# Attention, routing and eight experts on one Trainium2 core: zero products first, shorter routings, a new order on VectorE and ScalarE, and search tables of their own for two experts

## The reference, cut to what matters

```
attention   B=4, H=8, S=768, D=64; each chunk of 32 queries sees 16 keys to the left, its own 32,
            8 to the right and 8 memory keys; softmax over these 64; times the values
x           attention output as 3072 rows of 512
logits      x @ w_gate                      # 3072 x 8
routing     flat logits in descending order; a token goes to the expert of its largest logit whose
            count is still below cap = 384; so every expert gets exactly 384 tokens
for e in 8: h = relu(x[mask] @ w1[e]);  y[mask] = h @ w2[e]      # 512 -> 1024 -> 512
tail        z = y @ w_in (512 -> 1024); u = z * softmax(z); u centred, scaled by 1/std and g_ln;
            out = u @ w_out (1024 -> 512)
```

## Time and profile before

| | us |
|---|---|
| median of three runs | 782.75 |
| lowest and highest run | 779.54, 783.77 |
| the profiled execution | 780.36 |
| its span, first to last instruction | 778.6 |
| PE busy, share of the span | 704.8 (91%) |
| DVE / ACT / POOL busy | 541.3 / 327.2 / 314.7 |

### The profile page before, as it was taken

One profiled execution on the slowest core, in us unless ns is written; L12 is line 12 of the kernel. 1 busy time (PEld: TensorE's weight loads), 2 busy tenths in 40 slices (PEclk: granted clock), 3 DMA queues, 4 the chain that ended last, 5 costly groups with the idle time before them and its releaser, 6 DMA issues.

```text
span 778.6 us, 17877 instructions
## 1 busy us (share of the span) xinstructions
PE 704.8 (91%) x7092; PEld 626.8 (81%) x7093; DVE 541.3 (70%) x1957; ACT 327.2 (42%) x537; POOL 314.7 (40%) x241
## 2 busy tenths in 40 slices
PE   6799973299979999999999999999999999999992
PEld 5688862298878989798889898989898888889882
DVE  4376756887788688868886978688868877631240
ACT  1255536141365136513651474147315631572270
POOL 3011108582276138514751574158316821672011
PEclk9699985599999999999999999999999999999997
DMA  8699994340232033103310331033113301330001
GB/s 346 205 356 371 337 379 179 100 158 2 82 95 82 28 95 120 58 27 99 119 56 28 122 122 55 33 99 113 55 54 108 108 31 55 109 109 28 0 14 40
DMA packets 24924, 89.07 MB, mean 114 GB/s; under 512 B 3360, under 2 KB 3360, under 8 KB 24864
## 3 DMA queue, kind: packets, MB, share of 16 engines
q0 software_dynamic: 13056, 46.14, 18.0%
q1 hardware_dynamic: 11808, 42.17, 14.5%
HBM read 75.71 MB, written 12.58 MB: 113 GB/s over the span
## 4 chain that ended last, share of the span: by engine, by line
PE 67%; DVE 11%; POOL 8%; issue 5%; DMA 5%; ACT 3%; SPq 0%; POOLq 0%; DVEq 0%; ACTq 0%
PE banks L544 18%; PE banks L546 16%; PE banks L545 16%; POOL wl L1360 5%; DMA raw<-w,w_idx 4%; PE banks L475 3%; PE banks L432 3%; PE banks L456 3%; PE bank L442 2%; DVE z L1174 2%; PE bank L467 2%; POOL raw L1354 2%; PE banks L573 1%; PE banks L557 1%; DVE hits L995 1%
## 5 line engine op out<-in xcount | busy, mean ns | idle before, releaser
L1360 POOL TENSOR_TENSOR wl<-raw,wh 128x1024 fp32r<-128x1024 f32 x60 | 146.1, 2435 | 20.0 <-ACT wh L758 18.6
L1354 POOL DMA_INDIRECT raw<-w,w_idx x60 | 64.7, 1079 | 158.7 <-DVE w_idx L1089 121.5
L544 PE MATMUL banks<-xh,wh 128*128 128x384 f32 x256 | 90.9, 355 | 3.6 <-POOL wl L1360 3.4
L544 PE MATMUL banks<-hh,wh 128*128 128x384 f32 x256 | 90.5, 354 | 0.0
L546 PE MATMUL banks<-xh,wl 128*128 128x384 f32 x256 | 87.0, 340 | 0.0
L545 PE MATMUL banks<-xl,wh 128*128 128x384 f32 x256 | 86.8, 339 | 0.0
L546 PE MATMUL banks<-hh,wl 128*128 128x384 f32 x256 | 86.4, 338 | 0.0
L545 PE MATMUL banks<-hl,wh 128*128 128x384 f32 x256 | 86.3, 337 | 0.0
L758 ACT ACTIVATE wh<-raw 128x1024 fp32r<-128x1024 f32 x60 | 63.3, 1056 | 42.8 <-DMA raw<-w,w_idx 42.5
L544 PE MATMUL banks<-wout_h,uh 128*128 128x512 f32 x192 | 78.7, 410 | 0.2
L544 PE MATMUL banks<-win_h,yh 128*128 128x512 f32 x192 | 77.2, 402 | 0.0
(11 more groups left out here) (202 smaller groups left out, 1622.1 us busy)
## 6 DMA issues: line engine op xcount, KB each, us to landing
unit<-qk_in SPq DMA_DIRECT2D x24, 768.0 KB, 6.2
vr<-v_in SPq DMA_DIRECT2D x24, 520.0 KB, 5.0
x_rows<-x_keep SPq DMA_DIRECT2D x20, 256.0 KB, 5.0
prep_first<-w_in SPq DMA_DIRECT2D x4, 512.0 KB, 6.8
x_rows<-x_sb SPq DMA_DIRECT2D x4, 256.0 KB, 4.3
prep_first<-w_out SPq DMA_DIRECT2D x2, 512.0 KB, 8.8
prep_rest<-w_out SPq DMA_DIRECT2D x2, 512.0 KB, 10.2
raw<-w,w_idx POOLq DMA_INDIRECT x60, 4.2
```

The costliest lines, as they stand in the source:

```text
L544: nc.tensor.matmul(bank, stat_h, mov_h, start=first, stop=False)
L1354: gp.indirect_dma_start(stage(s, c), None, table, bass.IndirectOffsetOnAxis(ap=w_idx[:, c % WCH:c % WCH + 1], axis=0))\
L1360: gp.tensor_tensor(wl[:, c % WCH, :], stage(s, c), wh[:, c % WCH, :].bitcast(F32), ALU.subtract)\
```

## The change

It has five parts.

1. **Start.** SP issues unit 0 first and `wg` and `gain` behind it. TensorE multiplies a cleared 128x128 block with a cleared 128x512 block three times (`WARM`) before its loop, as soon as VectorE has cleared `pr[:, 1]`.
2. **Routing.** `place` is shortened for all experts: a scan that starts at 1000 and a triangular matrix with -1000 on its diagonal take the place of three operations; position and place are whole numbers, so that the third comes by a shift and the place by a mask. The work on `keep` and `M` goes into a new function `close` behind `write_ids`. `write_ids` is one reduction. For expert 0, positions are split in six spans of 64: `hot_b` has 1536 elements in place of 3072, and `token_ids` has 48 products in place of 24. `choose(0)` names the weight rows last, and the table `flips` is made inside the levels. Only six of the eight weight pieces are split ahead of expert 0; GpSimd makes the last two after expert 0's own weights.
3. **z stage on VectorE and TensorE.** The order is `choose, place, max_z(0), write_ids, close, best_open, weigh(0), max_z(1), begin_search, count, max_z(2), search, row_low`; for expert 0, `row_low` comes ahead of `max_z(2)`. TensorE takes `token_ids` after (3,1) and `best_T` after (5,0). ScalarE takes the exponential of z tile 0 one group earlier and its centring right behind it.
4. **h stage on ScalarE.** The last exponential, and the weight conversions 4 and 5, change places: the exponential of tile 2 comes in group 3, the conversions one group later, conversion 7 behind the last `uT_high`.
5. **Tables.** Two rounds instead of one are taken ahead of an expert's h groups; nothing stands at (7) of the first o group. Expert 0's and expert 1's searches have tables of their own, and VectorE's order (`COUNTS...`) is kept apart from TensorE's (`ROUNDS...`).

The diff, cut to its core:

```diff
-ROUNDS = rounds_of([[2]], [[2], [2], [3], [], [3], [3], [3], []], [[2, 7], [4]], [[0, 5], [2, 7], [4], [1, 6]])
-ROUNDS_FIRST = rounds_of([[0, 0]], [[2], [2], [2], [3], [3], [3], [3], [3]], [[], []], [[1, 5], [1, 5], [1, 5], [3]])
+ROUNDS = rounds_of([[0, 5]], [[2], [2], [3], [], [3], [3], [], [1]], [[2], [4]], [[0, 5], [2, 7], [4], [1, 6]])
+ROUNDS_FIRST = rounds_of([[0, 0]], [[2], [2], [2], [3], [3], [3], [3], [3]], [[], []], [[4], [1, 5], [1, 5], [1, 6]])
+ROUNDS_SECOND = rounds_of([[0]], [[], [2], [3], [], [3], [3], [], [1]], [[2], [0, 5]], [[0, 4], [1, 5], [1, 5], [1, 6]])
...
+COUNTS = rounds_of([[0, 5]], [[2], [2], [3], [], [3], [3], [3], []], [[2], [4]], [[0, 5], [2, 7], [4], [1, 6]])
...
+            pe.wait_ge(probs, 1)
+            blank = pr[:, 1, :, :, :].rearrange("p h a w -> p (h a w)")
+            for _ in range(WARM):
+                nc.tensor.matmul(PT_PS[:, :], blank[:, 0:P], blank, start=True, stop=True)
...
             def token_ids(f):
                 pe.wait_ge(hot_ready, f + 1)
+                parts = 2 if f == 0 else 1
+                wide = P // parts
                 for t in range(NT):
-                    mm = nc.tensor.matmul(TOT[:, 16:22], hot_b[:, t, :], rhs_id[:, t, :],
-                                          start=(t == 0), stop=(t == NT - 1))
+                    for a in range(parts):
+                        mm = nc.tensor.matmul(TOT[wide * a:wide * a + wide, 16:16 + 2 * TILES], hot_b[:, t, 0:wide],
+                                              rhs_id[:, t, TILES * a:TILES * a + TILES, :].rearrange("p i b -> p (i b)"),
+                                              start=(t == 0), stop=(t == NT - 1))
...
-                    if routed and (g, k) == (3, 3):
+                    if routed and (g, k) == (3, 1):
                         token_ids(s + 1)
-                    if routed and (g, k) == (5, 1):
+                    if routed and (g, k) == (5, 0):
                         best_T(s + 2)
...
             def place(f):
                 ve.wait_ge(ranks_ps, f + 1)
-                done(nc.vector.tensor_tensor_scan(upto[:, :], ones48[:, :], whole, 0.0, ALU.mult, ALU.add))
-                done(nc.vector.tensor_tensor(pos2[:, :], upto[:, :], whole, ALU.subtract))
-                done(nc.vector.tensor_tensor(pos2[:, :], pos2[:, :], within, ALU.add))
-                done(nc.vector.scalar_tensor_tensor(out=pos2[:, :], in0=picked[:, :], scalar=-MARK, in1=pos2[:, :],
-                                                    op0=ALU.mult, op1=ALU.add))
+                wide, spans, number = (HALF, 2 * TILES, iota_sixth) if f == 0 else (P, TILES, iota_third)
+                done(nc.vector.tensor_tensor_scan(upto[:, 1:], ones_f[:, 0:2 * NT], whole, MARK, ALU.mult, ALU.add))
+                done(nc.vector.tensor_tensor(pos2[:, :], upto[:, 0:2 * NT], within, ALU.add))
                 done(nc.vector.tensor_tensor(pos[:, :], pos2[:, 0:NT], pos2[:, NT:2 * NT], ALU.min))
...
+                nc.vector.tensor_scalar(pos_low[:, :], pos[:, :], wide - 1, None, ALU.bitwise_and)
+                done(nc.vector.tensor_scalar(pos_high[:, :], pos[:, :], wide.bit_length() - 1, None,
+                                             ALU.logical_shift_right))
...
+                nc.vector.tensor_tensor(hot_b[:, :, 0:wide], iota_low[:, 0:wide].unsqueeze(1).to_broadcast([P, NT, wide]),
+                                        pos_low[:, :].unsqueeze(2).to_broadcast([P, NT, wide]), ALU.is_equal)\
+                  .then_inc(hot_ready, 1)
...
+                choose(f)
+                place(f)
                 max_z(s, 0)
+                write_ids(f)
+                close(f)
+                best_open(f + 1)
+                weigh(s, 0)
                 max_z(s, 1)
...
-            for n in range(8):
+            def prepare_lo(n):
                 gp.wait_ge(prep_hi, n + 1)
                 gp.tensor_tensor(prep_low(n), prep_at[n], prep_high(n).bitcast(F32), ALU.subtract).then_inc(prep_lo, 1)
+
+            for n in range(6):
+                prepare_lo(n)
```

More of the change, by code:

```diff
@@ L686, in expert @@
                 if first:
-                    for _, j in ROUNDS[0][0]:
+                    for _, j in ahead:
                         total(s + 2, j)
@@ L1053, in first_search @@
                                                      shifted_int(SIXTEEN, -SIXTEEN_SHIFT), None, ALU.bitwise_xor))
+                    for j in range(SEARCH * n // LEVELS, SEARCH * (n + 1) // LEVELS):
+                        flip(j)
                     ve.wait_ge(level_ps, n + 1)
@@ L1154, in _ @@
             write_ids(0)
-            for j in range(SEARCH):
-                nc.vector.tensor_scalar(flips[:, j, :], digits[:, :], ROUND_SHIFT[j + 1] if j + 1 < SEARCH else 0,
-                                        shifted_int(FOUR, ROUND_SHIFT[j] - FOUR_SHIFT) if j else 0,
-                                        ALU.logical_shift_left, ALU.bitwise_xor)
+            close(0)
             best_open(1)
             begin_search(1)
-            search(1, ROUNDS_FIRST[0][0])
+            search(1, COUNTS_FIRST[0][0])
             def high(ap):
@@ L1224, in expert @@
                 f = s + 1
-                ahead, rh, ro, ry = rounds_in(first, last)
+                _, rh, ro, ry = counts_for(f)
                 for g in range(KF):
@@ L1256, in expert @@
                 y_low(s, KD - 1)
-                if not last:
-                    choose(f)
-                    place(f)
-                    write_ids(f)
-                    best_open(f + 1)
+                if last:
+                    max_z(s, 0)
+                    weigh(s, 0)
+                    max_z(s, 1)
+                    max_z(s, 2)
+                    return
+                choose(f)
+                place(f)
                 max_z(s, 0)
+                write_ids(f)
+                close(f)
+                best_open(f + 1)
+                weigh(s, 0)
                 max_z(s, 1)
-                if not last:
-                    begin_search(f + 1)
-                    count(f + 1, 0)
-                weigh(s, 0)
-                max_z(s, 2)
-                if not last:
-                    row_low(s + 1)
-                    search(f + 1, ROUNDS[0][0][1:])
+                begin_search(f + 1)
+                count(f + 1, 0)
+                ahead = counts_for(f + 1)[0][0][1:]
+                if first:
+                    row_low(s + 1)
+                    max_z(s, 2)
+                    search(f + 1, ahead)
+                else:
+                    max_z(s, 2)
+                    search(f + 1, ahead)
+                    row_low(s + 1)
             row_low(0)
@@ L1408, in expert @@
                         fetch_weights(s, c + 2)
-                if not first:
+                if first:
+                    for n in (6, 7):
+                        prepare_lo(n)
+                else:
                     rsqrt(s - 1)
```

153 lines of the change are left out of this document (86 added, 67 removed).

## The result

The changed kernel takes 760.7 us (median of 4, 759.47 to 761.49) against 782.0 us before; the ratio is 0.9737, interval 0.971 to 0.9765. Forecast were 757.5 us, range 749 to 766. The profiled execution took 760.91 us, its span is 759.1: 19.5 us less than before, where the parts of the forecast add up to 25.3. Where they come from is read between places that both timelines have: the starts of the first count product of the first level, of the last `digit`, of expert 0's `ids`, of the first h product (xh, wh) of each expert, and of the last output product.

What follows compares the result with a forecast made beforehand. TensorE, busy 704.8 us (91% of the span), was taken as the bound. Gains A to E of 4.0, 6.0, 3.1, 3.4 and 8.8 sum to 25.3 us: 780.4 to 755.1, with 757.5 forecast for the median, range 749 to 766.

Steps and rivals of the forecast that it cites:

- A: Kernel start: zero products raise TensorE's clock, first two steps faster, gaps unchanged; 4.0 us gained, bounds 0 and 8.9.
- Rival (2): Start: code comes in time once TensorE is warm and the clock stays up; 9.4 us more gained, 748; chance 0.08.
- B: Routing of expert 0: shorter naming, mask and place on VectorE; 6.0 us gained (4.7 to 6.9).
- the tables in the levels: Routing, in B: flips rows fit VectorE's waits inside the levels; cost 0.2 us if those were full.
- C: Expert 0's search, first y group: shorter wait for a count and no clock drop behind it; 3.1 us gained.
- D: Handover to expert 1: first h product waits less, clock may not fall; 3.4 us gained.
- the first fall of the clock: Expert 0, in C: half pace at 180 to 183 us goes with the idle stretch before it; 1.7 us gained.
- The second fall: Behind the handover wait, in D: clock may not fall with a shorter wait; 0.8 us, half of 1.7.
- E: Experts 1 to 6: ten TensorE waits for search counts largely go; 8.8 us gained (5.0 to 9.5).
- (1): Waits move instead of going: E gives a third, 3 us, and D half; 765; chance 0.16.
- (3): Whole-number compares in hot_b take twice as long per element, 6.7 us; slower kernel, 791; chance 0.03.
- (4): Start: zero products don't raise the clock; A is -0.4, time 761.9; chance 0.10.

Runs made afterwards that it cites:

- experiment 2: Changed kernel without the zero products (WARM = 0): 759.0 us, ratio 0.9742 to the kernel before.
- 1: Changed kernel measured again with no edit, as base on the same chip: 759.4 us, ratio 0.974 to the kernel before.
- experiment 11: Kernel of experiment 10 without the zero products (WARM = 0): 753.5 us, ratio 0.967 to the kernel before.
- experiment 10: Changed kernel plus five edits: flips before levels, five weight pieces ahead, loads held back, later y-group rounds on TensorE, earlier ScalarE high halves: 754.0 us, ratio 0.9675.
- experiment 7: Changed kernel with expert 0's old search table and z tile 2's maximum back ahead of the low halves: expert 0 takes 59.19 us, 1.9 more.
- experiment 8: Kernel before with only part 4 of the change (h stage on ScalarE): 772.9 us in a single execution, against 780.2.
- Experiment 9: Kernel before with one more search round ahead of the h groups and none at (7) of the first o group: 796.9 us in a single execution.
- experiment 4: Changed kernel with the whole flips table made before the levels instead of inside them: 760.0 us, ratio 0.9741 to the kernel before.

## Why the prediction was right, and where it was wrong

**A, wrong.** I took 4.0 us; the measured value is 0 within about 2 us (experiment 2 against 1; experiment 11 against 10, also within 0.1%, is less sharp). The step that failed is the choice within the bounds: "the first steps' gain with the gaps as they are". The bound that stood beside it was what happened: the code comes no sooner, and what two fast steps win is given back at the next stop, where the clock is lost again too. I had counted the two stops that the trace showed, and not asked for a third: at 11.87 a faster TensorE reaches the end of its code, which a slow one reached after it had arrived. With and without the zero products work goes on at 21.3 to 21.7 us. Where the code does come sooner (experiment 10 against 11) the gain is lost to the clock instead. The end of the lower level behind that was at 34.4 and at 41.3 us for the same code (27.2 to 44.6 over all kernels), and the first level product moved by 3.5 us with it. What sets this point wasn't found. Rival (2) fell too: with the loads as they are, no packet of code came sooner for the raised clock. The second gap is shorter than the 2.13 us of the first trace (0.80), but so it is without the zero products (1.28).

**B, right in sum, one part unseen.** Last digit to `ids` gained 7.4, more than the 6.0: the naming left the path and `e_hot`, held for 0.91 us before, is free (0.22), which I had not counted. I had put the last digit just ahead of 132.6 us; it stands at 131.06, and `e_hot` lies between. `token_ids` costs 0.65 in place of 1.1: its products start 27 ns apart in both kernels, so the narrower weights cost nothing more per product. But the tables in the levels cost 3.15 us in the first trace and 2.6 in the second, where I had written 0.2 "if those were full". They were full: VectorE waits 0.56 us in a level, and two rows take 0.8 while GpSimd works. In the last one they are held by a whole product of GpSimd. I had read that mechanism from the earlier trace rows for `w_idx` and `mask` and didn't apply it to the rows that the change puts beside the same products. I had quoted only half of the rule as well. The same section of the Trainium skill (“SBUF — State Buffer”, “Who interferes with whom”) names copies, casts and tensor-scalar instructions next to those with two SBUF inputs, where they run in a two-port mode, but not tensor-scalar with an accumulator and not reductions. The traces agree with each: `flips`, `e_hot` and `w_idx` (tensor-scalar) were held, while a reduction (`e_star`, 0.15 us) and a row of one element (`e_rows`, 0.15) beside the same product, and the counts with their accumulator (0.48), were not.

**C and D, right in sum, with clock terms whose reason failed.** The count's wait went from 1.88 to 0.32 us (1.6; forecast 1.4). TensorE's idle time at the handover went from 3.35 to 1.83, and 0.88 us of waiting inside the transposes went as well (2.4; forecast 2.6). That is 4.0 of the 6.1 us; the first fall of the clock, taken at 1.7, makes most of the rest. It is there in all three traces of kernels built on the one before and in none of the eleven built on the changed one. But I had hung it on the wait, and experiment 7 has the wait without the fall; what removed it isn't known. The second fall lies in expert 1: it is there in the same three traces, and in two of the eight traces of the changed kernel and its near variants. Expert 1 takes 76.4 us with it and 74.9 without.

**E, right in size, half wrong in cause.** Experts 1 to 6 gained 9.7 us; forecast 8.8. I gave the wait of the seventh h group to ScalarE's conversion (shown in 8) and the other to the round taken ahead. Experiment 9 shows that the round does remove it, at the price of a longer one in the third o group, and 8 that ScalarE's part removes it without that price. Part of the 9.7 is no wait at all: expert 1 before holds the second fall of the clock, which I had counted in D. The last term, expert 7, has the same cause (87.48 in experiment 8) and wasn't in my sum: 1.6 us.

**The rivals.** (1) waits that move: in part they did. A new wait in the first y group of experts 1 to 6 costs 0.4 to 0.7 us each; it came with ScalarE's part (experiment 8 has it alone), and experiment 10 took it away. (3), slower compares: `hot_b` 3.35 us, no. (4), no rise of the clock: the clock rose, and the time was as if it hadn't. So the median missed by 3.2 us and the sum of the parts by 5.8 (19.5 us in the profiled pair, not 25.3). On one side stand A, 4 us and another 2 by which this trace's start is later, and the levels' 3.2; on the other B's 1.4, E's 0.9 and expert 7's 1.6. That the total came so near is in part luck: gains that I had not counted stand against a term of 4 us that brought nothing.

## What to carry to other kernels

When a stall caused by another engine is taken off one instruction, look which instruction of the same kind stands next in that stretch; only work that leaves the stretch, or the other engine's work moved out of it, ends the stall (both were needed here: experiment 4 gained 1.1 to 1.7 us of 3.1, experiment 10 all of it). A gain of pace in a kernel's first microseconds counts only up to the next stop for code or data, so ask for each such stop when a faster engine would reach it, and whether the clock is still up behind it. And where a start differs by 3 us between executions of the same code, cut the trace at fixed places and compare the stretches, not the totals.

## What the runs showed of the hardware

- A VectorE tensor-scalar of 4 to 8 elements a partition whose operands lie in SBUF took 0.9 to 2.3 us beside a weight product of GpSimd, ending with it (`e_hot` 133.00 + 1.67 against 129.99 + 4.66); operations that write a PSUM bank beside the same products stayed at 0.17 us, and search counts (L1023) at 0.48.
- In the first round of its loop TensorE stopped two or three times where it waited for no semaphore, at fixed places of its stream, and went on 2.2 to 2.6 us after a packet of its instruction queue had started, in all fourteen traces. With the loads held back the second packet started at 16.25 to 17.32 us with the zero products (18.26 to 19.35 with the loads as they are) and at 18.36 without them (18.81 to 18.99).
- The granted clock fell for 3.4 us behind a handover wait of 1.8 us in two of nine traces, and not behind one of 2.5 us in another: the same wait can cost 1.5 us more or nothing.
- At the start the granted clock stood at the lower level while TensorE was busy for 21.34 of 25 us (15 to 40 us, the changed kernel). The same code had the upper level back at 34.4 us in another execution and at 41.3 in this one.
- `weigh`, a VectorE instruction with both tensors in SBUF, took 2.61 us where a product of GpSimd had started first, and 1.21 where it started first itself; the product then took 3.11 in place of 2.40 us (experiment 8).
